# Second MLP: products 1 and 2 leave PSUM by ScalarE, and VectorE adds them from SBUF

## The reference, cut to what matters

```
def _moe2_ref(x, w_gate, w_val, w_out) -> np.ndarray:   # x 1536x512, w_gate and w_val 512x1536, w_out 1536x512
    g = x @ w_gate
    silu = g * (1.0 / (1.0 + np.exp(-g)))
    val = x @ w_val
    return (silu * val @ w_out).astype(np.float32)
```

## Time and profile before

| | before |
|---|---|
| median of 3 runs | 780.21 us (780.07 to 780.3) |
| the profiled execution | 779.8 us |
| its span, first to last instruction | 778.0 us |
| mean granted TensorE clock | 1.000 |
| busy: PE, PEld | 773.2 us (99%), 700.5 us (90%) |
| busy: DVE, ACT, POOL | 569.0 (73%), 516.3 (66%), 523.1 us (67%) |

### The profile page before, as it was taken

The page is one execution under the profiler, slowest core; times in us unless marked ns, Lnnn a source line. Parts: engine busy times, 40 slices in busy tenths (PEclk is TensorE's granted clock), DMA queues, the critical chain, the costliest instruction groups (busy, mean ns, idle before and its releaser), DMA issues.

```text
span 778.0 us, 12682 instructions
## 1 busy us (share of the span) xinstructions
PE 773.2 (99%) x4231; PEld 700.5 (90%) x4231; DVE 569.0 (73%) x1046; ACT 516.3 (66%) x960; POOL 523.1 (67%) x457
## 2 busy tenths in 40 slices
PE   9999999999999999999999999999999999999998
PEld 8999999999998888888888888899999999999997
DVE  6999999999998787777777777644544555554554
ACT  7888888888888787686777789553554444333322
POOL 4878999998575997222222488879888975665610
PEclk9999999999999999999999999999999999999999
DMA  8857665463402600000000111341212214211002
GB/s 189 196 138 183 166 175 139 118 163 90 121 14 82 190 0 1 1 0 1 1 0 1 29 44 38 95 122 55 55 28 55 55 29 134 55 42 41 27 1 82
DMA packets 57521, 57.53 MB, mean 74 GB/s; under 512 B 6576, under 2 KB 44272, under 8 KB 57456
## 3 DMA queue, kind: packets, MB, share of 16 engines
q1 hardware_dynamic: 57296, 56.32, 26.9%
q10 hardware_dynamic: 160, 0.39, 0.2%
HBM read 33.59 MB, written 3.15 MB: 47 GB/s over the span
## 4 chain that ended last, share of the span: by engine, by line
PE 98%; DVE 1%; issue 0%; ACT 0%; POOL 0%; POOLq 0%
PE ps L1310 19%; PE ps L1311 19%; PE ps L1312 19%; PE ps L1464 8%; PE ps L1481 4%; PE ps L1408 4%; PE ps L1409 4%; PE ps L1483 4%; PE ps L1407 4%; PE ps L1445 4%; PE ps L1450 4%; PE ps L1515 2%; PE ps L1306 1%; DVE neg_max L1191 1%; DVE probT_lo L1217 0%; PE ps L1419 0%
## 5 line engine op out<-in xcount | busy, mean ns | idle before, releaser
L599 POOL TENSOR_TENSOR den<-den,mag 128x512 f32<-128x512 f32 x48 | 62.4, 1300 | 120.1 <-ACT den L780 119.9
L1312 PE MATMUL ps<-x_hi,w_lo 128*128 128x512 f32 (+1 forms) x384 | 139.5, 363 | 0.0
L658 POOL TENSOR_TENSOR w_lo<-w_raw,w_hi 128x768 fp32r<-128x768 f32 (+1 forms) x48 | 101.6, 2125 | 56.3 <-ACT w_hi L839 56.3
L1310 PE MATMUL ps<-x_hi,w_hi 128*128 128x512 f32 (+1 forms) x384 | 139.4, 363 | 0.0
L1311 PE MATMUL ps<-x_lo,w_hi 128*128 128x512 f32 (+1 forms) x384 | 139.4, 363 | 0.0
L680 POOL TENSOR_SCALAR prob<-prob,row_inv 128x768 f32<-128x768 f32 x96 | 85.9, 912 | 28.0 <-DVE row_inv L1207 27.1
L1217 DVE TENSOR_TENSOR probT_lo<-ps,probT_hi 128x384 fp32r<-128x384 f32 x192 | 97.3, 548 | 6.1 <-ACT probT_hi L927 5.1
L927 ACT ACTIVATE probT_hi<-ps 128x384 fp32r<-128x384 f32 x192 | 83.7, 489 | 22.7 <-PE ps L1464 21.4
L1191 DVE TENSOR_REDUCE neg_max<-ps 128x1 f32<-128x768 f32 x96 | 90.9, 948 | 1.1 <-PE ps L1450 0.8
L907 ACT ACTIVATE prob<-ps,neg_max 128x768 f32<-128x768 f32 x96 | 86.7, 904 | 2.9 <-DVE neg_max L1191 2.7
L1464 PE MATMUL ps<-ident,prob 128*128 128x128 f32 x576 | 79.8, 274 | 0.2
(11 more groups left out here) (150 smaller groups left out, 1988.8 us busy)
## 6 DMA issues: line engine op xcount, KB each, us to landing
w_raw<-in_moe_w_gate SPq DMA_DIRECT2D x48, 128.0 KB, 2.3
w_raw<-in_moe_w_val SPq DMA_DIRECT2D x48, 128.0 KB, 2.6
k_hihi<-qk_hi SPq DMA_DIRECT2D x31, 192.0 KB, 3.3
w_raw<-in_moe_w_in SPq DMA_DIRECT2D x16, 256.0 KB, 3.5
w_raw<-in_moe_w_out SPq DMA_DIRECT2D x16, 256.0 KB, 4.5
qk_raw<-in_q SPq DMA_DIRECT2D x16, 192.0 KB, 4.0
qk_low<-qk_hi SPq DMA_DIRECT2D x16, 192.0 KB, 3.7
qk_low<-qk_lo SPq DMA_DIRECT2D x16, 192.0 KB, 4.1
```

The lines of the kernel that those rows point to most:

```text
L658: did(g.tensor_tensor(lo[:, wave, :], raw[:, wave, :], hi[:, wave, :].bitcast(F32), ALU.subtract), s_w2lo)
L1310: mm(dst, hi, m_hi, start=start, stop=False)
L1312: return mm(dst, lo, m_hi, start=False, stop=stop)
```

## The change

In every unit but the first (m >= 1), a new function `keep_parts` on ACT, directly after `first_part`, copies product 1 from PSUM to the tile `gate_1` and product 2 to the tile `sum_3`, both of them free at that time. DVE's `sum_two` and `gate_zero` then read these two tiles in place of the banks, so that both inputs of both additions lie in SBUF. PE's block 3 waits for the first copy (`s_kept_1`) in place of `s_sum_2`, and block 4 for the second (`s_kept_2`) in place of `s_gate_0`. The addition into `sum_3` gets one more wait, for `s_gate_0`, because `gate_zero` reads that tile first.

```
@@ ScalarE
+            def keep_parts(m):
+                sc.wait_ge(s_part[1], m + 1)
+                sc.wait_ge(s_prod, 2 * m)
+                s.activation(gate_1[:, :], ps[:, banks(m)[1], 0:TH], ACT.Copy).then_inc(s_kept_1, 1)
+                sc.wait_ge(s_part[2], m + 1)
+                sc.wait_ge(s_val_1, m)
+                s.activation(sum_3[:, :], ps[:, banks(m)[0], 0:TH], ACT.Copy).then_inc(s_kept_2, 1)
@@ ScalarE, mlp2
                 if m:
                     first_part(m)
+                    keep_parts(m)
                 if m == 1:
@@ VectorE, sum_two
-                ve.wait_ge(s_part[1], m + 1)
-                v_.tensor_tensor(sum_2[:, :], ps[:, banks(m)[1], 0:TH], gate_0[:, :], ALU.add
-                                 ).then_inc(s_sum_2, 1)
+                if m:
+                    ve.wait_ge(s_kept_1, m)
+                else:
+                    ve.wait_ge(s_part[1], 1)
+                part_1 = gate_1[:, :] if m else ps[:, banks(m)[1], 0:TH]
+                v_.tensor_tensor(sum_2[:, :], part_1, gate_0[:, :], ALU.add).then_inc(s_sum_2, 1)
@@ VectorE, gate_zero
-                v_.tensor_tensor(gate_0[:, :], ps[:, banks(m)[0], 0:TH], gate_0[:, :], ALU.add
-                                 ).then_inc(s_gate_0, 1)
+                part_2 = sum_3[:, :] if m else ps[:, banks(m)[0], 0:TH]
+                v_.tensor_tensor(gate_0[:, :], part_2, gate_0[:, :], ALU.add).then_inc(s_gate_0, 1)
@@ VectorE, mlp2
                 ve.wait_ge(s_sum_2, m + 1)
+                ve.wait_ge(s_gate_0, m + 1)
                 v_.tensor_tensor(sum_3[:, :], two, sum_2[:, :], ALU.add).then_inc(s_sum_3, 1)
@@ TensorE, part
-                    pe.wait_ge(s_sum_2, m + 1)
+                    if m:
+                        pe.wait_ge(s_kept_1, m)
+                    else:
+                        pe.wait_ge(s_sum_2, 1)
                 elif k == 4:
-                    pe.wait_ge(s_gate_0, m + 1)
+                    if m:
+                        pe.wait_ge(s_kept_2, m)
+                    else:
+                        pe.wait_ge(s_gate_0, 1)
```

## The result

| | before | after |
|---|---|---|
| median | 780.14 us (6 runs, 780.0 to 780.3) | 785.59 us (6 runs, 785.33 to 786.02) |
| ratio of the fast runs | | 1.0071, 95% interval 1.0061 to 1.0081 |
| profiled execution's span | 778.0 us | 784.1 us |
| busy ACT | 516.3 us, 960 instructions | 536.9 us, 1006 instructions |
| busy DVE | 569.0 us | 573.0 us |

What follows compares the result with a forecast made beforehand. PE's own stream was taken to bound the kernel (98% of the chain). Terms 0.8 + 1.8 + 0.6 + 0.5 + 0.6 + 1.0 = 5.3, less 0.4, gave +4.9 on 780.21: 785.1 us, range 781.0 to 788.0.

Steps and rivals of the forecast that it cites:

- Step 2: ACT's copies delay w_hi, making POOL 2.0 us late; blocks 0 and 1 of unit 4 wait, PE loses 1.7 us once.
- Step 3: DVE additions with two SBUF inputs and POOL operations exclude each other, in order of arrival: nothing to +3.6 us.
- Units 5 to 11: POOL's round grows to 11.59 us against PE's 11.47, so seven units lose 0.12 each: +0.8 to +1.0 us.
- Step 1: Blocks 3 and 4 are freed sooner, gaining 0 to 0.9 us; half taken, -0.4, as sum_3 uses block 5's spare time.
- Units 12 to 23: POOL has finished its sums before product 1 is there and waits for w_hi: no loss.
- POOL and DVE not disturbing each other: Rival: no exclusion on SBUF, leaving the late POOL's +1.7 less 0.4, +1.3, 781.5 us; chance 0.25.
- POOL keeping SBUF over back-to-back operations: Rival: DVE gets in only at a POOL pause, some 3 us more in units 2 and 3, 788 us; chance 0.1.
- An absorbed `w_hi`: Rival: ACT's late w_hi costs PE nothing, leaving a gain of 0.9 us at best, 779.3 us; chance 0.08.
- the one row that I had for the exclusion: DVE's 128x4 SBUF TENSOR_SCALAR took 0.28 us, its 128x2 twin 0.16; ended at 231.34, a POOL operation at 231.32.

Runs made afterwards that it cites:

- the copies alone: Kernel before plus two ACT copies per unit, on idle SBUF data that nobody waits for, behind products 1 and 2: 782.09 us against 780.08, ratio 1.0024.
- the run from unit 2 on: Changed kernel, but unit 1 too takes products 1 and 2 as before, so only units 2 to 23 are changed: 783.85 us, ratio 1.0048.
- the own tile: Changed kernel, but product 2 is copied to a tile of its own, so sum_3 need not wait for gate_zero: 782.48 us, ratio 1.0029.
- the two probes: Kernel before plus one short unused DVE operation behind gate_zero, units 13 to 23: a two-input SBUF addition or a one-input maximum; spans 778.3 and 778.5 us.
- the probe with one input: Kernel before plus an unused DVE maximum over 128 SBUF columns behind gate_zero, units 13 to 23: 0.28 us in all eleven, span 778.5 us.

## Why the prediction was right, and where it was not

The forecast, 785.1, lies 0.5 us from the 785.59 measured, and the sign and the two mechanisms named for it are shown. That the total came so close is luck, since terms with errors of up to 1.7 us offset each other. Point by point:

- **Step 2, POOL late behind ACT's copies: right.** Forecast 2.0 us late and 1.7 us on PE if it stood alone; 1.9 late in the rows, and 1.6 us on PE by the rows with the copies alone.
- **Step 3, exclusion of DVE and POOL: right in kind, too large in units 2 to 4.** Forecast for these units with step 2 in it: 0.8 + 1.8 + 0.6 + 0.5 + 0.6 = 4.3 us; measured 0.29 + 1.60 + 1.01 = 2.9. In the order of the forecast's terms these are 0.29 in unit 2 (for 0.8), 1.28 at block 5 of unit 3 (for 1.8), 0.32 and 0.56 at blocks 0 and 1 of unit 4 (for 0.6 and 0.5), and 0.46 at its block 5 (for 0.6). Of the 2.9, 1.6 are step 2's by the run with the copies alone, and 3 x 0.11 the loss of each unit, which leaves about 1.0 for the exclusion; the run from unit 2 on has the same 1.4 without step 2. The term mis-sized is the overlap: in unit 2 `sum_two` and `gate_zero` stood 0.22 and 0.19 us (0.78 and 0.75 for 0.56) where I had 0.6 and 0.75, in unit 3 0.09 and 1.17 where I had 0.45 and 1.85. POOL was 0.1 us less late and DVE asked 0.05 later than I had taken, and each shortened wait also took less time from POOL: its last weight sum of unit 3 ended 2.9 us late (539.27, less 0.66, for 535.76), where I had 4.0.
- **Units 5 to 11: nearly the right sum, wrong cause.** I had 1.0 us from POOL's round of 11.59 us. They lost 0.11 each, 0.8 in all, but units with an idle POOL lose just as much; with the own tile they take 11.44 to 11.48 for the 11.43 of later units, so the exclusion costs them some 0.03 us a unit.
- **Step 1: wrong in sign.** I took `gate_zero` and `sum_3` to use 0.1 of the 0.11 us that block 5 had to spare, and booked a gain of 0.4. The chain grew by more than twice that: 0.05 for the second wait ahead of `gate_zero`, and 0.08 between `gate_zero` and `sum_3` (0.69 for 0.61). Block 5 lost 0.11 us in each unit. The gain for blocks 3 and 4 was there, 0.04 us a unit; the own tile lays it bare. My reading of where it comes from was off: a block's length ends with the start of the next, so the 0.02 us above 1.04 belong to the starts of blocks 4 and 5. Nor is it shown that they come from a late release, since with `gate_zero` 0.07 us sooner and nothing else changed the two blocks together took as long as before. That stays open.
- **Units 12 to 23: forecast nothing, lost 1.1 + 0.45 + 0.14.** That is the same 0.11 a unit, and 0.35 in unit 22 alone. There `sum_3` started 1.04 to 1.07 us behind `gate_zero` in place of 0.69, in all three kernels in which it waits for `gate_zero` and the additions have their double wait, and in none without one of the two. Why it is this unit stays open.
- **The rivals.** POOL and DVE not disturbing each other falls with the two probes. POOL keeping SBUF over back-to-back operations falls too: in unit 3 `gate_zero` went ahead as soon as L636 had ended, and POOL's next operation stood behind it. An absorbed `w_hi` falls with the copies alone. What the earlier trace rows showed, the one row that I had for the exclusion, the probes leave open: it has a single SBUF input, and the probe with one input was not held.

So the forecast had 1.4 us too much in units 2 to 4 and 0.2 in units 5 to 11. It had 2.2 us too little: 0.4 of gain that didn't come out, 0.1 in unit 1 and 1.7 from unit 12 on, where the late block 5 was booked at nothing. The difference is the 0.5 us, but for rounding. The range would have held without their offsetting each other; the hit to within 0.5 us would not.

With the rule of the Trainium skill that the prediction named (SBUF — State Buffer, Who interferes with whom) the traces agree: 0.67 us for 0.28 with two SBUF inputs, 0.28 with one. The table of the Trainium skill in VectorE: DVE Perf Modes (The TRN2 errata) gives an operation from SBUF 58 cycles of fixed cost and one from PSUM 120. Here an addition of 384 columns takes 0.56 us from SBUF alone, and as much from PSUM and SBUF, so the measurement decides against a gain from that.

## What to carry to other kernels

Moving an operand from PSUM to SBUF is no local edit: a two-input VectorE operation that read only SBUF stood here behind each GpSimd operation that it met, all of which read SBUF too, and the wait hid in its duration, not in idle time. When a hand-over gets one more step, add up the whole chain to the next block that waits for it, waits included, and compare it with the hundredths that are to spare; a wait that has long been met was 0.06 us here, in each of 23 units, and taking it out gave 1.4 us where the chain was late and nothing where it was not. And a copy that itself delays nobody can still delay what is queued behind it on its engine. A place where the engine has a pause may be better; no run here tried one.

## What the runs showed of the hardware

- A second wait ahead of a VectorE operation cost 0.06 us even when it had been met (0.10 against 0.04 us from the end of the copy). With three waits, `sum_3` followed 0.69 us behind the start of the operation that it depended on; elsewhere, with two waits, the distance is 0.60 (655.60 to 656.20 in unit 13 of the changed kernel). No run took one of the three away, so that the third wait makes the difference is not shown.
- A VectorE operation with two SBUF inputs waited for GpSimd's to end (0.67 us for 0.28, ending 0.15 us behind it); one with a single SBUF input didn't.
- In the exclusion POOL pays as well: a weight sum of 0.74 us showed 1.05 where a VectorE addition went first.
- A block of matmuls released late by about 0.1 us showed no idle time at all, only a first matmul of 0.44 us in place of 0.33 and a distance of 0.28 us to the second in place of 0.17.
